# Attention's loads in another order, and the first weight stage on ScalarE's DMA queue

## What is computed

```
for t in range(768):                                  # attention, per batch and head
    m_new  = maximum(f_gate[t] + m, i_gate[t])
    f_stab = exp(f_gate[t] + m - m_new); i_stab = exp(i_gate[t] - m_new); m = m_new
    C = f_stab * C + i_stab * outer(v[t], k[t])
    n = f_stab * n + i_stab * k[t]
    y[t] = sigmoid(o_gate[t]) * (C @ q[t]) / maximum(abs(n . q[t]), 1)
x = y as [1536, 320]
h = x @ w_in;  x = maximum(0.01 * h, h) @ w_out       # dense layer
P = softmax-like gates of x @ w_gate, eight rounds of norms
out = sum over e of P[:, e] * (relu(x @ w1[e]) @ w2[e])
```

## Time and profile before

| | us |
|---|---|
| median of three runs | 1006.07 (1004.85 to 1007.33) |
| the profiled execution | 1007.05 |
| its span in the trace | 1005.3 |
| TensorE busy | 978.7 (97%) |
| VectorE, ScalarE, GpSimd busy | 411.3, 296.5, 72.6 |
| attention's units and the prologue, up to | about 112 |
| bytes read from HBM | 36.91 MB |

### The profile page before, as it was taken

One profiled execution on the slowest core, in us unless ns is written; L12 is line 12 of the kernel. 1 busy time (PEld: TensorE's weight loads), 2 busy tenths in 40 slices (PEclk: granted clock), 3 DMA queues, 4 the chain that ended last, 5 costly groups with the idle time before them and its releaser, 6 DMA issues.

```text
span 1005.3 us, 14926 instructions
## 1 busy us (share of the span) xinstructions
PE 978.7 (97%) x5397; PEld 864.4 (86%) x5408; DVE 411.3 (41%) x784; ACT 296.5 (29%) x553; POOL 72.6 (7%) x146
## 2 busy tenths in 40 slices
PE   7699999999999979999999999999999999999998
PEld 5689988888778869998899999989998999899887
DVE  4546755546543364234244233324423332442222
ACT  4456444434432321123122121212212121321111
POOL 4335200000000322000000000000000000000000
PEclk9989999999999999999999999999999999999999
DMA  9774300210030002003001200300210030000000
GB/s 115 164 107 61 115 1 1 67 48 1 1 115 1 1 23 94 1 0 115 1 0 32 83 1 0 115 0 0 64 51 0 0 115 0 0 0 0 26 26 26
DMA packets 68462, 39.47 MB, mean 39 GB/s; under 512 B 52496, under 2 KB 64560, under 8 KB 68432
## 3 DMA queue, kind: packets, MB, share of 16 engines
q1 hardware_dynamic: 68256, 38.98, 16.3%
q10 hardware_dynamic: 176, 0.10, 0.0%
HBM read 36.91 MB, written 1.97 MB: 39 GB/s over the span
## 4 chain that ended last, share of the span: by engine, by line
PE 93%; SPq 4%; DVE 1%; DMA 1%; issue 0%; ACT 0%; DVEq 0%
PE psA L1108 44%; PE psB L1146 11%; PE psB L1148 11%; PE psB L1147 11%; PE psB L1124 2%; PE psB L1126 2%; PE psB L1125 2%; PE psB L1026 2%; PE psA L1003 1%; PE psB L1131 1%; PE psB L1130 1%; PE psA L996 1%; PE psB L1013 1%; SPq L288 1%; PE psB L1038 1%; SPq L328 1%
## 5 line engine op out<-in xcount | busy, mean ns | idle before, releaser
L659 ACT ACTIVATE gh<-psA 128x512 fp32r<-128x512 f32 x192 | 114.9, 598 | 538.1 <-PE psA L1108 538.1
L885 DVE SCALAR_TENSOR_TENSOR gl<-psA,gh 128x512 fp32r<-128x512 f32 x192 | 132.9, 692 | 340.9 <-ACT gh L659 340.7
L1146 PE MATMUL psB<-w2s,gh 128*128 128x320 f32 x768 | 237.6, 309 | 0.0
L1147 PE MATMUL psB<-w2s,gh 128*128 128x320 f32 x768 | 237.3, 309 | 0.0
L1148 PE MATMUL psB<-w2s,gl 128*128 128x320 f32 x768 | 237.2, 309 | 0.0
L1108 PE MATMUL psA<-xh,w1h 128*128 (+1 forms) x480 | 190.5, 397 | 0.0
L1108 PE MATMUL psA<-xl,w1h 128*128 (+1 forms) x480 | 189.8, 395 | 0.0
L1108 PE MATMUL psA<-xh,w1l 128*128 (+1 forms) x480 | 189.1, 394 | 0.0
L1147 PEld LDWEIGHTS psB<-w2s,gh 128*128 128x128 f32 x768 | 144.3, 188 | 5.5
L1146 PEld LDWEIGHTS psB<-w2s,gh 128*128 128x128 f32 x768 | 144.2, 188 | 5.1
L1148 PEld LDWEIGHTS psB<-w2s,gl 128*128 128x128 f32 x768 | 144.4, 188 | 0.0
(11 more groups left out here) (150 smaller groups left out, 878.6 us busy)
## 6 DMA issues: line engine op xcount, KB each, us to landing
raw<-in_moe_w_dram SPq DMA_DIRECT2D x16, 640.0 KB, 8.3
raw<-in_moe_w_dram SPq DMA_DIRECT2D x8, 1024.0 KB, 5.3
raw<-in_moe_w_dram SPq DMA_DIRECT2D x16, 256.0 KB, 6.1
raw<-in_moe_w_out_dram SPq DMA_DIRECT2D x4, 640.0 KB, 9.3
raw<-in_moe_w_in_dram SPq DMA_DIRECT2D x2, 1024.0 KB, 6.0
qs<-in_q_dram SPq DMA_DIRECT2D x12, 160.0 KB, 3.3
ks<-in_k_dram SPq DMA_DIRECT2D x12, 160.0 KB, 4.0
vz<-in_v_dram SPq DMA_DIRECT2D x24, 80.0 KB, 3.8
```

Source lines behind the costliest of these rows:

```text
L659: act.activation(gh[:, f % RING, :], h_ps[:, f % HB, :], ACT.Relu).then_inc(ghi_ok, 1)
L885: dve.scalar_tensor_tensor(out=gl[:, f % RING, :], in0=h_ps[:, f % HB, :], scalar=0.0, in1=gh[:, f % RING, :].bitcast(F32), op0=ALU.max, o ...
L1146: pe.matmul(bank, gh[:, slot, cols], W2S[par][:, f, 0, :], start=first, stop=False)
L1147: pe.matmul(bank, gh[:, slot, cols], W2S[par][:, f, 1, :], start=False, stop=False)
```

## The change

It has five parts. (1) The first stage's five loads are issued by ScalarE, after the copies of unit 1 and ahead of the first sigmoid, and no longer by SP ahead of unit 4. (2) SP waits for `cm` before it issues q and k of unit 1; the first four output-gate loads come in two halves around the rows of units 0 and 1, and v of unit 1 after the rows. (3) For units 2 and 3 and in the loop from unit 4 on, the rows are issued right behind q and k of their unit and ahead of its v; units 2 and 3 no longer have all their loads ahead of all their rows. (4) Behind each sigmoid ScalarE takes the exponential of one zero per partition, `exp_again`, which nobody reads; the exponential's table is loaded there. (5) TensorE runs 9 warm-up matmuls for 6 ahead of unit 0's exponents, and 7 more behind them.

```
+        def stage_parts(eng, w1_src, w2_src):
+            eng.dma_start(raw1[:, 0:KT, :], w1_src[0:KT * P, :].rearrange("(t p) f -> p t f", p=P)).then_inc(raw_in, 16)
+            eng.dma_start(raw1[0:DR, KT, :], w1_src[KT * P:DM, :]).then_inc(raw_in, 16)
+            eng.dma_start(raw1[DR:P, KT, :], w1_src[KT * P:DM, :]).then_inc(raw_in, 16)
+            w2_v = w2_src.rearrange("(f p) d -> p f d", p=P)
+            eng.dma_start(raw2[:, 0:NF // 2, :], w2_v[:, 0:NF // 2, :]).then_inc(raw_in, 16)
+            eng.dma_start(raw2[:, NF // 2:NF, :], w2_v[:, NF // 2:NF, :]).then_inc(raw_in, 16)
...
-            def load_gates_out(i):
-                for j in range(U_IT):
+            def load_gates_out(i, units=range(U_IT)):
+                for j in units:
...
             load_v(0)
-            load_gates_out(0)
+            sp.wait_ge(m_in, 16)
             load_qk(1)
-            load_v(1)
+            load_gates_out(0, range(B))
...
             expo_rows(sp, 0, (-1, PARTS - 1))
             expo_load(1)
-            for n in range(2, U_IT):
-                load_qk(n)
-                load_v(n)
-            for n in range(2, U_IT):
-                expo_load(n)
+            load_gates_out(0, range(B, U_IT))
+            load_v(1)
+            load_qk(2)
+            expo_load(2)
+            load_v(2)
+            load_qk(3)
+            expo_load(3)
+            load_v(3)
             load_gates_out(1)
...
-            load_stage(0, w_in[:, 0:FW], w_out[0:FW, :])
             for n in range(U_IT, NU):
...
                 load_qk(n)
+                expo_load(n)
                 load_v(n)
-                expo_load(n)
...
                 act.activation(tile, tile, ACT.Sigmoid).then_inc(sig_done, 1)
+                act.activation(exp_again[:], zero1[:], ACT.Exp)
...
             qk_copies(0, 1)
+            stage_parts(act, w_in[:, 0:FW], w_out[0:FW, :])
             out_gates(0)
...
-            warm(6)
+            warm(9)
             exponents(0, 0)
+            warm(7)
```

More of the change, by code:

```diff
@@ L136, in build @@
         zero1 = asb("zero1", [P, 1], F32)
+        exp_again = asb("exp_again", [P, 1], F32)
         rw_t = asb("rw_t", [P, 2, BH * NC], F32)
@@ L351, in load_stage @@
                 at_least(sp, w_ready, PIECES * s)
[L352 to L357, removed]
+                stage_parts(sp, w1_src, w2_src)
             load_qk(0)
```

## The result

The changed kernel takes 1000.77 us (median of five executions, 998.64 to 1001.87) against 1006.4 before; the ratio is 0.9941 with a 95% interval of 0.9924 to 0.9959. The gain is 5.6 us, half of the 11.1 forecast; the time lies 0.2 us inside the stated range of 991.5 to 1001. The execution with the trace took 999.02 with a span of 997.3, which is 8.0 less than the span of before. Between the first matmul of the dense layer and the end nothing changed: that matmul started at 113.02 and starts at 104.95, 8.1 earlier, and the span is 8.0 shorter.

The account below looks back on a forecast made before the run. TensorE was taken as the bound (93% of the chain), with only attention's waits for rows and the low clock behind them to win. Unit 4 8.9 us earlier plus 2.2 at full clock gave 11.1: 1006.07 to 995.0 us, range 991.5 to 1001.

Parts of the forecast that it names:

- The prologue: Before unit 1: cm lands sooner as SP waits for it, gain 1.1 us (0 to 1.8); unit 0 at about 14.8.
- rival (d): Eight loop units: SP becomes the bound, rows waiting ahead of v and v's issue meeting a full queue; 1016 us, chance 0.04.
- The five issues: ScalarE, between unit 1's copies and the first sigmoid: issuing the stage takes 2.5 to 4.7 us, 2.9 taken.
- (b): Rival: ScalarE hangs in its stage issues, exponential(2) at most 37.5, gain 4.8 us, 1001.2 us; chance 0.20.
- The 1.4 us for the clock: Before scores(1) end: warm-up matmuls fill the stretch preceding the low clock, regaining 1.4 us (0 to 1.7).
- at nothing, then: Prologue: ten extra warm-ups lie within waits of 1.22 and 1.86 us and cost nothing; without that cover up to 2.5.
- which makes 22.3 and with 1.5 us to land 23.8: SP's issues ahead of unit 2: its rows land at 23.8, so the 1.82 us wait goes and t2 is 24.3.
- t4 = 43.3: Start of unit 4's exponents' matmuls, after the engines move the stage and ten tensors; 52.19 before, 8.9 us gained.
- then runs at full clock, 7.27 instead of 9.50: Unit 4 on TensorE: no low clock after the stall, 2.2 us more gained.
- Rival (a): Stage fits in the gaps small tensors leave: t4 = 40.4, t5 = 47.6, gain 14.1 us, 992.0 us; chance 0.17.
- t5: Start of unit 5's exponents' matmuls on TensorE, where gains are summed: 50.6 forecast against 61.69, 11.1 us gained.
- Rival (c): Stall only moves: stage starves SP's small packets, 13.5 us ahead of unit 3 or 4; 1004 us, chance 0.07.

Follow-up runs that it names:

- the other traces: The changed kernel, unaltered, measured twice more for a second and third trace: 1001.49 and 1001.40 us.
- paced kernel: Changed kernel with the first stage issued by ScalarE in three groups, behind the exponentials of units 2, 4 and 6, instead of all at once: 994.79 us.

## Why the prediction was right in its direction and wrong by half in its size

**What held.** The bound: attention's waits for rows, and nothing after attention; all of it shifted as one. The prologue: `cm` came in 2.35 us, a gain of 1.7 near the upper bound of 0 to 1.8 (1.1 was taken), unit 0 at 14.35, and 15.17 and 15.26 in the other traces (14.8 forecast), the end of scores(1) at 23.63, 24.44 and 24.53 (24.3). The loop units: 7.24 us from unit 5 to 6 (53.38 to 60.62), SP no bound, rival (d) nowhere. The second table load and the one-element exponential (0.20 us, as estimated) cost nothing visible. ScalarE's exponential of unit 2 started at 28.87 (28.3 forecast). The five issues took it 4.3 us, in the range of 2.5 to 4.7 and above the 2.9 taken; the rows came later still, so that was hidden. One of them took 1.86 us, more than the 1.5 that was to be a sign of (b); it took 1.52 with almost nothing to move, and (b)'s chain, exponential(2) at up to 37.5, didn't come.

**What held by luck.** The 1.4 us for the clock came, but not from the warm-up matmuls that were to fill the stretch: without them scores(1) ended at 23.63 and the clock was 1.00 as well. The warm-ups also weren't "at nothing, then": `cm` coming sooner took away the wait that was to cover the first three. And that the median lies inside the range is luck. It does so by 0.2 us, two more executions, 1001.49 and 1001.40, lie outside, and the way there wasn't the one forecast.

**What failed first: unit 2.** The step was "which makes 22.3 and with 1.5 us to land 23.8". The issues did end at 22.2; the rows landed at 27.8. The working had the stage's first byte at 22.5, since ScalarE "was free at 23.07" in the trace before, and so kept unit 2's rows out of the reckoning of transfers. But the issue didn't wait for ScalarE's copies to end; the stage was issued from 19.22, beside the rows (19.21 to 22.22). With the stage on SP again unit 2 began at 24.03, which shows the rest of the step to be sound. Being issued first isn't what decides: with the stage from 25.34 on, unit 3's rows, issued from 24.32 to 27.16, were waited for until 33.42. Cost: 3.5 us of start, and behind the wait 2.0 us of unit 2 at half clock (9.28 instead of 7.27), for which the forecast had only a place in its range.

**What failed second: unit 4.** "t4 = 43.3" was made of bytes: stage and ten tensors at the engines' rates. Measured 46.43, and 47.26 and 47.18 in the other traces. By bytes it would even be earlier, as the stage began 3 us sooner. Of the 3.1 us, 1.2 came from unit 2: scores(3) ended at 46.43 - 1.93 = 44.50. The other 1.9 are the wait. The windows show the engines far from busy by then: share 0.29 at 34 to 36 and 0.25 at 40 to 42 us. The last wait is SP's queue itself: it hung until 30.68 on k of unit 3, and from there to the end of unit 4's rows at 45.33 its timeline has one issue after another (rows 3, v, four output gates, three gate weights, q, k, rows 4: 14.6 us). Without the stage's traffic that same issue of k took 0.59 us. The forecast priced the hang nowhere but in rivals (b), on ScalarE's side, and (d), in the later units, and took SP's time per unit, 5.15, as cover only.

**The third, in the medians alone:** unit 4 "then runs at full clock, 7.27 instead of 9.50". In the first trace it took 6.95, in the others 8.59 and 8.59, at the lower clock, behind a wait of 3.60 and 2.65 us.

**In sum** at unit 5: forecast 50.6, first trace 53.38, others 55.8. The gain there is 8.3 or 5.9, of 11.1. Rival (a), 992.0, is near what the kernel does without the stage's traffic (993.92, with unit 0 2.3 later); by the traces this traffic is worth 7.0 to 8.6 us. Rival (b) was the wrong queue: ScalarE wasn't what hung, though its t5 of 56.8 and 1001.2 us lie close to the later traces. Rival (c) came nearest in its mechanism: the stage did starve SP's small packets, but ahead of unit 2, and for 4.19 us and 1.93 more ahead of unit 4 instead of 13.5. (The sum of (d) takes off (a)'s 14.1; with the forecast's own 11.1 it would be 12.7 lost and not 9.7.)

The Trainium skill's page DMA: Bandwidth & Descriptors, section Issuing engines are not separate DMA queues, says that transfers issued by different engines interleave on the same 16 DMA engines. The runs agree: q1 moved 0.48 MB in 11 us beside q10's 2.41, and the stage moved alone gave 3.3 us of the median, the stall having gone from unit 4 to unit 2.

## What to carry to other kernels

A block of loads taken out of one queue and put into another is still in the way of everything small that is issued while it moves: look for what is due in that stretch, and split the block by when its parts are first needed. Here that was worth 6.0 us in the medians, about as much again as the whole change. ScalarE's DMA issue started when its list reached it, 1.6 us before the copies ahead of it had ended, so the time of an issue is to be read from the waits ahead of it, not from the engine's busy rows. And a queue's time is to be summed twice, once in bytes and once in issues behind its longest hang; ahead of unit 4 the second was the later.

## What the runs showed of the hardware

SP's issue of a 160 KB load (1024 runs of 160 B) hung 6.23 us in the changed kernel while ScalarE's stage moved, though the stage was no longer in SP's queue; with the stage issued later four such issues took 11.61 us. Without the stage's traffic the same issue took 0.59. `cm`, 48 KB, took 2.35 us while SP issued nothing, 4.03 and 4.70 while it issued loads beside it. None of TensorE's waits of 1.43, 1.81, 1.93 and 2.52 us ahead of a unit (paced kernel, first trace of the changed one) was followed by a lower clock; in the changed kernel's three traces all five of 2.65 to 4.19 us were, and each fall cost the unit behind it 1.6 to 2.3 us against the 6.95 of unit 4 at full clock. The extra warm-up matmuls made no difference to the clock of unit 1 in the two traces without them; why it had been at 1.2 GHz in the trace before the change stays open. What the traces show beside it is the waits ahead of units 0 and 1: 1.22 and 1.86 us before the change, 1.21 and 1.87 with only the stage moved, where the clock was 0.50 at 20 to 22 us as well, but 0.19 and 1.65, and 0.70 and 1.60, in the two without warm-ups.
